# A fused delta-rule attention, Sinkhorn MoE and routed MoE kernel: the order of loads, copies and norm parts within a step, and the start of expert 1

## The reference

```python
# attention: q, k, v are (4, 8, 768, 48), beta (4, 8, 768)
k_n = k / (norm(k) + 1e-6)
for t in range(S):
    y[t] = q[t] @ state
    state = state + beta[t] * outer(k_n[t], v[t] - state.T @ k_n[t])
# first MoE on x (3072, 384), 8 experts, 1024 hidden: Sinkhorn weights
P = exp(x @ w_gate - max)
for _ in range(8):
    P /= P.sum(1) + 1e-9; P /= P.sum(0) + 1e-9; P *= N / E
x2 = sum over e of P[:, e] * (relu(x @ w1[e]) @ w2[e])
# second MoE: one expert for each token, by the largest cosine to an
# expert's embedding, weighted by the softmax of the cosines / tau
out = gate * (relu(x2 @ v1[idx]) @ v2[idx])
```

## Time and profile before

| | us |
|---|---|
| median of 3 runs | 2307.51 |
| lowest and highest | 2306.09 and 2309.39 |
| the profiled execution, its own time | 2312.33 |
| its span | 2310.5 |
| TensorE busy in it | 2216.6 (96%) |
| VectorE busy | 1016.1 (44%) |
| ScalarE busy | 600.1 (26%) |
| GpSimd busy | 97.1 (4%) |
| mean granted TensorE clock | 0.965 of full speed |

### The profile page before, as it was taken

One profiled execution on the slowest core, in us unless ns is written; L12 is line 12 of the kernel. 1 busy time (PEld: TensorE's weight loads), 2 busy tenths in 40 slices (PEclk: granted clock), 3 DMA queues, 4 the chain that ended last, 5 costly groups with the idle time before them and its releaser, 6 DMA issues.

```text
span 2310.5 us, 42613 instructions
## 1 busy us (share of the span) xinstructions
PE 2216.6 (96%) x17911; PEld 2056.3 (89%) x17911; DVE 1016.1 (44%) x1882; ACT 600.1 (26%) x1016; POOL 97.1 (4%) x91
## 2 busy tenths in 40 slices
PE   5889999999999999999999999999999999699998
PEld 5888898998999999899899989989999998699998
DVE  7575465345333333323333232323323234767764
ACT  2232222331111111111111111111111122366664
POOL 0000000000000000000000000000000000122221
PEclk6699999999999999999999999999999999699999
DMA  8544434331000000000000000000000011566662
GB/s 314 152 136 135 132 116 122 98 131 55 1 28 1 28 1 29 28 1 28 1 28 1 28 28 1 28 1 28 1 1 1 1 42 42 196 250 239 232 236 72
DMA packets 152504, 172.69 MB, mean 75 GB/s; under 512 B 81580, under 2 KB 112464, under 8 KB 152338
## 3 DMA queue, kind: packets, MB, share of 16 engines
q1 hardware_dynamic: 143090, 158.70, 21.2%
q0 software_dynamic: 3968, 10.82, 1.2%
q10 hardware_dynamic: 5280, 0.66, 0.2%
HBM read 144.19 MB, written 27.33 MB: 74 GB/s over the span
## 4 chain that ended last, share of the span: by engine, by line
PE 89%; DVE 5%; DMA 2%; issue 2%; ACT 1%; SPq 1%; POOL 0%; ACTq 0%; POOLq 0%; DVEq 0%
PE psA L1689 21%; PE psH L1704 15%; PE psB L1689 8%; PE psB L1704 8%; PE psY L1704 7%; PE psY L1829 6%; PE psH L1582 4%; PE psY L1597 4%; PE psA L1463 4%; PE psB L1815 3%; PE psA L1815 3%; PE psB L1555 1%; DVE products L1040 1%; DVE sx L1043 1%; PE psB L1565 1%
## 5 line engine op out<-in xcount | busy, mean ns | idle before, releaser
L1689 PE MATMUL psA<-X,wh 128*128 128x512 f32 x1440 | 450.6, 394 | 5.8 <-DVE wl L1192 4.1
L1199 DVE SCALAR_TENSOR_TENSOR hl<-psA,hh 128x512 fp32r<-128x512 f32 x240 | 166.1, 692 | 629.5 <-ACT hh L840 629.4
L840 ACT ACTIVATE hh<-psA 128x512 fp32r<-128x512 f32 x240 | 143.8, 599 | 836.9 <-PE psA L1689 836.9
L1689 PEld LDWEIGHTS psA<-X,wh 128*128 128x128 f32 x1440 | 266.6, 188 | 51.8 <-issue 7.4
L1689 PE MATMUL psA<-X,wl 128*128 128x512 f32 x720 | 285.4, 396 | 0.0
L1704 PE MATMUL psH<-wh,hh 128*128 128x384 f32 x672 | 228.3, 340 | 0.0
L1704 PE MATMUL psH<-wh,hl 128*128 128x384 f32 x672 | 227.2, 338 | 0.0
L1704 PE MATMUL psH<-wl,hh 128*128 128x384 f32 x672 | 225.8, 336 | 0.0
L1199 DVE SCALAR_TENSOR_TENSOR hl<-psB,hh 128x512 fp32r<-128x512 f32 x96 | 66.5, 693 | 277.2 <-ACT hh L840 277.2
L1689 PE MATMUL psB<-X,wh 128*128 128x512 f32 x576 | 179.2, 392 | 0.0
L1423 DVE TENSOR_TENSOR vl<-vs,vh 128x768 fp32r<-128x768 f32 x152 | 145.7, 962 | 56.3 <-ACT vh L885 55.6
(11 more groups left out here) (281 smaller groups left out, 4152.3 us busy)
## 6 DMA issues: line engine op xcount, KB each, us to landing
vs<-v_d SPq DMA_DIRECT2D x38, 768.0 KB, 6.5
vs<-v_d SPq DMA_DIRECT2D x19, 1536.0 KB, 12.4
ws<-w_d SPq DMA_DIRECT2D x28, 768.0 KB, 6.0
kT<-kT_d SPq DMA_DIRECT2D x17, 512.0 KB, 4.2
qT<-qT_d SPq DMA_DIRECT2D x15, 512.0 KB, 5.1
a_scratch<-an SPq DMA_DIRECT2D x12, 512.0 KB, 3.8
kq<-kn_d SPq DMA_DIRECT2D x6, 768.0 KB, 6.9
vn<-vn_d SPq DMA_DIRECT2D x12, 384.0 KB, 4.4
```

Source lines behind the costliest of these rows:

```text
L840: act.activation(hh[kk % 3][:, :], ps_h[kk % (2 if last else 3)], ACT.Relu).then_inc(hh_ready, 1)
L1199: dve.scalar_tensor_tensor(hl[b][:, :], ps_h[bank], 0.0, hh[b][:, :].bitcast(F32), ALU.max, ALU.subtract).then_inc(hl_ready, 1)
L1689: mm = pe.matmul(to, a[half][:, c, col], X[:, 2 * g:2 * g + 2, b, c, :], start=(n == 0), stop=(n == 3 * KC - 1))
```

## The change

SyncE: within a step, the loads of the shared keys kTs and queries qTs come ahead of load_blocks and store_inverse. VectorE: within a step, the pm copy, then scale and values, come ahead of norms, reduce_part and mask. Norm parts: part 3 is a batch of its own (32 columns, norms(3) in step 11, root(3) in step 10); parts 4 and 5 are a batch of 64 columns, with squares in steps 24 and 25, reductions in 25 and 26, root(4) in step 26 and norms(4) in step 27. ScalarE's high_x waits for all reductions from chunk 4 on only. The embedding norm moves from steps 18 and 19 to 22 and 23. Units 0 and 1: both halves of y0s are copied by ScalarE. Expert 1: VectorE makes the layer 1 low part in step 101, where it did a Sinkhorn half; the later halves follow one place later (halves_done is 7 instead of 8). TensorE's hidden waits for the layer 1 low part alone, and give, in the first sub-step of each half of an expert, for that of layer 2.

```diff
-BATCH_ENDS = [1, 2, 3, PARTS]
+BATCH_ENDS = [1, 2, 3, 4, PARTS]
...
-AT_PART = [None] * 3 + [9, 10, 11]
+AT_PART = [None] * 3 + [9, 24, 25]
+AT_NORMS = {AT_PART[3] + 2: 3, AT_PART[5] + 2: 4}
...
-AT_EMB = 18
+AT_EMB = 22
 SPILLED = 10
+
+UNITS_ALONE = 2
...
-                    if s == 12:
-                        load_blocks(2)
-                    if s in range(24, 16 * NG - 24, 16):
-                        load_blocks(s // 16 + 2)
-                    if s - 1 in AT_SOLVED:
-                        store_inverse(AT_SOLVED.index(s - 1))
                     if s - 1 in AT_KS[1:NC - 1]:
                         c = AT_KS.index(s - 1)
                         sp.wait_ge(ks_done, c)
...
                             sp.wait_ge(m_done, c + 5)
                             sp.dma_start(qTs[:, :, :], qT[c]).then_inc(s_qT, 16)
                         sp.dma_start(kTs[:, :, :], kT[c + 1]).then_inc(s_kT, 16)
+                    if s == 12:
+                        load_blocks(2)
+                    if s in range(24, 16 * NG - 24, 16):
+                        load_blocks(s // 16 + 2)
+                    if s - 1 in AT_SOLVED:
+                        store_inverse(AT_SOLVED.index(s - 1))
...
                     if c >= 2:
                         act.wait_ge(g_done, 6)
+                    if c >= 4:
                         act.wait_ge(s_red, PARTS)
...
                     act.activation(to, ps_u[0], ACT.Copy).then_inc(y0a_ready, 1)
+                    if u < UNITS_ALONE:
+                        act.activation(y0s[:, 1, :], ps_u[1], ACT.Copy).then_inc(y0b_ready, 1)
...
-                    if s == AT_PART[-1] + 1:
-                        root(3)
+                    if s + 1 in AT_NORMS:
+                        root(AT_NORMS[s + 1])
...
                     u = unit_after(s)
-                    if u is not None:
+                    if u is not None and u >= UNITS_ALONE:
                         unit_out(u)
                     k = block_of(s)
                     if k is not None:
                         low(k)
+                    if s in AT_SC:
+                        c = AT_SC.index(s)
+                        dve.wait_ge(sc_done, c + 1)
+                        dve.tensor_copy(pm[:, ST * c:ST * (c + 1), :], ps_sc.rearrange("p (t e) -> p t e", t=ST)).then_inc(sc_ready, 1)
+                    if s - 1 in AT_GRAM:
+                        scale(AT_GRAM.index(s - 1), psA)
+                    if s in AT_KS:
+                        values(AT_KS.index(s))
                     if s == AT_SPLIT_END + 1:
                         norms(2)
                     if s - 1 in AT_PART:
                         reduce_part(AT_PART.index(s - 1))
-                    if s == AT_PART[-1] + 2:
-                        norms(3)
-                    if s - 1 in AT_GRAM:
-                        scale(AT_GRAM.index(s - 1), psA)
-                    if s in AT_KS:
-                        values(AT_KS.index(s))
+                    if s in AT_NORMS:
+                        norms(AT_NORMS[s])
                     if s in AT_MASK:
                         mask(AT_MASK.index(s))
-                    if s in AT_SC:
-                        c = AT_SC.index(s)
-                        dve.wait_ge(sc_done, c + 1)
-                        dve.tensor_copy(pm[:, ST * c:ST * (c + 1), :], ps_sc.rearrange("p (t e) -> p t e", t=ST)).then_inc(sc_ready, 1)
...
-                    if s >= first_iteration:
+                    if s >= first_iteration and s != LAST - 1:
                         sinkhorn_half(s - first_iteration)
-                halves_done = LAST - first_iteration
+                    if s == LAST - 1:
+                        split1(1, 0)
+                halves_done = LAST - 1 - first_iteration
                 unit_out(NC - 1)
...
-                split(1, 0)
+                split2(1, 0)
                 expert(1, False)
...
                     if kk % (STEPS // 2) == 0:
-                        pe.wait_ge(wh_ready, 2 * (2 * (e - 1) + half + 1))
-                        pe.wait_ge(wl_ready, 2 * (2 * (e - 1) + half + 1))
+                        pe.wait_ge(wl_ready, 2 * (2 * (e - 1) + half) + 1)
...
                     pe.wait_ge(hl_ready, k + 1)
+                    if kk % (STEPS // 2) == 0:
+                        pe.wait_ge(wl_ready, 2 * (2 * (e - 1) + half) + 2)
```

More of the change, by code:

```diff
@@ L1120, in _, with split1 @@
                 reduce_part(0)
+                def split1(e, half):
+                    H = 2 * (e - 1) + half
+                    dve.wait_ge(wh_ready, 2 * H + 1)
+                    dve.tensor_tensor(wl1[half][:, :, :], ws1[half][:, :, :], wh1[half][:, :, :].bitcast(F32), ALU.subtract).then_inc(wl_ready, 1)
                 dve.wait_ge(s_beta, 16)
@@ L1181, in _, with split2 @@
                         dve.wait_ge(sk_exp, 1)
-                    if s >= first_iteration:
+                    if s >= first_iteration and s != LAST - 1:
                         sinkhorn_half(s - first_iteration)
-                halves_done = LAST - first_iteration
+                    if s == LAST - 1:
+                        split1(1, 0)
+                halves_done = LAST - 1 - first_iteration
                 unit_out(NC - 1)
                 def split(e, half):
+                    split1(e, half)
+                    split2(e, half)
+                def split2(e, half):
                     H = 2 * (e - 1) + half
-                    dve.wait_ge(wh_ready, 2 * H + 1)
-                    dve.tensor_tensor(wl1[half][:, :, :], ws1[half][:, :, :], wh1[half][:, :, :].bitcast(F32), ALU.subtract).then_inc(wl_ready, 1)
                     dve.wait_ge(wh_ready, 2 * H + 2)
```

## The result

| | before | changed |
|---|---|---|
| median of the timed runs, us | 2306.80 (4 runs) | 2285.21 (4 runs) |
| lowest and highest | 2304.66, 2309.39 | 2276.90, 2289.73 |
| the profiled execution, its own time | 2312.33 | 2289.73 |
| its span | 2310.5 | 2287.9 |
| mean granted TensorE clock | 0.965 | 0.972 |

The changed kernel takes 0.9890 of the time of before (95% interval 0.9870 to 0.9909), 21.6 us less by the medians, whose quotient is 0.9906. The prediction was 32.5 us less. Between the two profiled executions the difference is 22.6 us, and the trace lets it be booked by stretch.

A forecast was written before the change was run, and what follows sets the result against it. TensorE was taken to set the end, losing time in pauses and the lower clock behind them. Terms 6.3 + 6.3 + 7.5 + 6.9 - 0.8 + 6.3 = 32.5 us, from 2307.51 to 2275 us; range 2268 to 2290 us.

The forecast's parts named there:

- Queries in steps 40 and 56: Before outputs(5) and outputs(7): qT issued earlier removes pauses of 3.86 and 3.99 us; gain 6.3 us each.
- What is passed: SyncE, steps 24, 40, 56: sa copies and inverse stores now stand behind the loads' waits; cover 1 us on SyncE.
- What comes back: Steps 24 to 27: moved norm work delays the pm copy, so cross(4) waits; 0.8 us charged, ends 0 and 5 us.
- Keys in step 12: Before gram(6): kT no longer behind eight sa copies, its 1.54 us pause goes; counted in the 7.5 us distance.
- Units 0 and 1, norm parts: corner(2) to outputs(2): y0s wait of 2.63 us goes, norms(3) shrinks; 7.5 us gained with the keys, ends 5 and 8.2.
- Step 20: Before cross(3): embedding norm and mask leave the pm copy's front; gain 7.2 us less 0.3 for unit 1, 6.9 us.
- Expert 1: Start needs only layer 1's wl: 3.4 us earlier, first nine matmuls faster, acc wait gone; 6.3 us, ends 3.4 and 6.3.
- The signs: Trace marks: right, no qT, kT waits, cross(4) under 1.2 us; wrong, st wait at keys_state(4), r_scratch issued after sr is ready.
- Rival 1: Short pauses left around step 14, at cross(4) and before expert 1 drop the clock: 10 us less gain, 2285 us; chance 0.21.
- Rival 2: Queries still late because their load runs beside the sa copies: both 6.3 us fall away, 2287.5 us; chance 0.11.
- Rival 4: Slower: SyncE's sa copies and inverse store become last in steps 24, 40, 56, needing over 2 us per copy; chance 0.04.

The follow-up runs named there:

- g1: The changed kernel itself, unedited, run a second time: 2286.61 us, ratio 0.9888 to the kernel before.
- h1: The changed kernel itself, unedited, run a third time: 2286.83 us, ratio 0.9908 to the kernel before.
- e1: The kernel before with only SyncE's new order of issues: 2302.86 us against 2309.92, ratio 0.9973.
- e3: The kernel before with only the new start of expert 1: 2304.22 us, ratio 0.9971.
- g3: The changed kernel with norm parts 3 to 5 in one batch again, squares in steps 9 to 11: 2295.10 us, one execution.
- h3: The changed kernel with units 0 and 1 copied by both VectorE and ScalarE again: 2300.27 us, one execution.
- g4: The changed kernel with only the embedding norm back in steps 18 and 19: 2290.64 us, one execution.
- g2: The changed kernel with odd-chunk inverse reloads five steps later, unit 6 on ScalarE alone, sixteenth Sinkhorn half in sub-step 3: 2279.88 us, ratio 0.9862.
- h2: The same kernel as g2, run again beside the changed kernel: 2277.23 us, ratio 0.9861 to the kernel before.
- e4: The changed kernel with SyncE's six reloads of the odd chunk's inverse five steps later: 2281.60 us, ratio 0.9875 to the kernel before.
- h4: The changed kernel with only the pm copy back behind the mask: 2287.85 us, one execution.
- e2: The kernel before with the change's VectorE and ScalarE parts, but SyncE's old order and expert 1's old start: 2300.45 us, ratio 0.9968.

## Why the prediction came out as it did

The sign, the kind of loss (a pause plus the clock behind it) and the range held: 2285.2 us lies in 2268 to 2290. The central 2275 us was 10 us too low. Where a term below is met to 0.1 us, it is met in one pair of executions. By its own steps:

- **Queries in steps 40 and 56**: right in place and size. outputs(4) to keys_state(6) and outputs(6) to keys_state(8) fell by 6.3 us each, as priced. The failed step stands beside it, in "What is passed": it counted what stands behind the loads in steps 24, 40 and 56 and found a cover of 1 us on SyncE. It did not count what those delay one step later. It took the twelve reloads in steps 25, 41 and 57 as fixed and never asked when the kn, qT and kT issues behind them come, nor that a TensorE made some 15 us earlier (206.66 to 191.13) would ask for kT before SyncE is there. And it let the r_scratch store land as fast as before. "What comes back" held the pm copy alone, 0.8 us. In its place: 12.8 us in the stretches of gram(8) and gram(10), 11.4 us in g1, and 3.2 in h1, which had lost its time in steps 13 to 16 already. Forecast 32.5 less these further 12.0 is 20.5 us, measured 22.6.
- **Keys in step 12**: the wait is gone (134.04). By itself it brought nothing that can be told from scatter (in e1 keys_state(2) to outputs(2) took 30.89 us, in the kernel before and e3 32.91 and 29.67), since y0s was next; its gain needs the units on ScalarE. That the sa copies "do not come later" failed: the last of the eight issues ends 8.4 us after keys_state(2) (133.14), 6.3 us after it in the kernel before, and VectorE, which is early now, stands waiting.
- **Units 0 and 1, norm parts**: the sum was met (corner(2) to outputs(2) 15.46 us against 23.03: 7.6 us, forecast 7.5), but partly by luck: the same stretch took 19.79 us in e3, still the kernel before there, and 17.32 and 19.52 in g1 and h1. The reason within it was wrong. I put it down to norms(3); g3 shows no gain of the smaller batch, and h3 shows that it is the unit copies, in one execution each. Neither wait of 0.3 us charged for ScalarE's copies is there. But "scale(6), which write_values(2) waits for, comes about when TensorE is there, so nothing more is lost" failed: the wait is 1.14, 1.92 and 1.97 us in the three profiles of the changed kernel.
- **Step 20**: right. outputs(2) to keys_state(4) fell by 6.9 us, and no pause stands before cross(3). g4 shows the embedding norm's share as 4.2 us, in one execution.
- **What comes back**, the pm copy at cross(4): 0.77 us, forecast 0.8. "state(3) is there just as keys_state(4) asks" was a little short: a wait of 0.63 us, 0.82 in g1, 1.83 at the low clock in h1.
- **Expert 1**: right in kind. The start came 0.85 us behind the last unit copy and the first nine matmuls at full clock; keys_state(8) to the end gave 2.8 + 4.4 = 7.2 us against 6.3.
- **The signs.** All that it named for being right came in this execution. Two that it named for being wrong came too: TensorE waits on st at keys_state(4), and near step 24 SyncE issues r_scratch 1.6 us after sr is ready. The second points at the queue that did cost the time.
- **The rivals.** Neither of the two at 2285 and 2287.5 us happened as written. Rival 1 has the right time mostly for another reason: in the profiled execution its short pauses (0.77, 0.85, 1.14 us) left the clock alone, and the clock fell behind pauses of 2.7 and 3.4 us that it did not name. In h1 a part of it is seen: VectorE late in steps 13 to 16, and the clock down behind scale(6). Rival 2's queries were on time. Rival 4 looked on the right queue for the right reason, but put the loss at the store, and its bound of 2 us per sa copy was not needed: SyncE was late behind the store, by 5 us. In its working "three times 13 us or so" should be three times 11 (12.6 less the slack of 4, plus 2.4), which is the 33 us it starts from.

## What to carry to other kernels

When loads are moved to the front of a queue, follow that queue to the next load the bounding engine asks for, and compare its issue with the moment that engine will come after the change, not before. A load that goes 0.4 us after its release is a wait that is covered by luck: every microsecond won upstream uncovers it. Where a gain passes on, look for the cheapest thing on the same queue that nobody needs yet (here half of the reloads) and move that back, here by five steps; it was worth as much as the largest of the three parts. Look at every step in which the same block of issues stands: here it held up two kinds of load, kT and sa. And take more than one profile before a stretch is booked to a us: two executions of one program differed by 4 us in one stretch of 26.

## What the runs showed of the hardware

**A store behind other traffic.** The time from issue to landing of the same store to r_scratch near step 24 is shorter where SyncE had issued nothing for a while before it. With 0.05 us or less it landed in 5.4 to 5.9 us (the changed kernel, g1, g2, g3, h1, h2, e4) and once in 4.2 us (h4); with 0.4 us in 4.0 us (e2), with 0.6 us in 3.3 us (e1), with 1.4 us in 2.7 us (g4), with 1.6 us in 2.9 us (before), with 4.4 us in 2.6 us (h3). Counted from the end of the issue in front, it is 3.9 to 5.9 us in all but h3 (7.1): a store handed over earlier landed hardly earlier. It does not hold as a size elsewhere: near steps 40 and 56 the same store, 0.05 us behind the issue in front, landed in 5.4 and 3.7 us (the changed kernel), 3.9 and 3.8 us (e1), 3.8 and 3.7 us (h2). The Trainium skill ("DMA: Bandwidth & Descriptors", section on queues, rings and completion order) says that a transfer's completion is counted only after every earlier write of the same DMA engine, across its queues. The trace fits that and does not test it; which of the transfers in front decides was not tried.

**The clock does not go by the length of a pause.** It stayed at full level behind pauses of 1.92 us (g1), 2.08 us (g3, 147.97: the 64 matmuls take 2.07 us) and 2.43 us (e3, for y0s at 144.54, with a granted clock of 1.00 from 144.5 to 152). It fell behind 1.34 us (g4: 3.15 us for 64 that take 2.08), 1.90 us (h4) and, at the very place of g1's 1.92, behind 1.97 us (h1: 3.65 us for 64 that take 2.07). In g4 it even fell behind pauses of 0.78 and 0.30 us in a row (207.33: 3.44 us), with a granted clock of 1.00 from 195 to 207. Between 110 and 560 us of these profiles every single pause of 2.5 us or more was followed by the low level. So my reading "1.5 us or more costs 2 to 4 us on top, 1 us costs itself" can't be kept: up to 2.4 us the length does not tell. The rule of the Trainium skill that the prediction quotes ("TensorE: Matmul & The Clock Gate", Part 1), that it matters where a pause falls, agrees with that. The Trainium skill says it of where the first matmul falls, and the prediction carried it over to pauses; no run here sets where a pause falls.

**VectorE beside GpSimd.** The mask of 128x1024 took 1.22 us in h4, where it started before GpSimd's product, and 2.16 us (the kernel before) and 2.31 us (g4) where it started 1.0 and 0.25 us after it. Both of these ended 1.1 us after GpSimd's product did (176.32 against 175.24, and 170.38 against 169.30).

What stays open: why executions of one program differ by up to 6 us before outputs(1), and by 4 us between keys_state(2) and outputs(2).
